# Two attention-and-MLP stages on one core: from three attention visits per unit to one, in one unrolled program

## The chip, the core and the metric

The kernel runs on one NeuronCore of a Trainium2 chip. Its engines are PE (TensorE, the matrix engine), DVE (VectorE), ACT (ScalarE), POOL (GpSimd) and SP (SyncE, which here only issues transfers). The metric is the device time in microseconds (us) of one execution; lower is better.

## The reference: what is computed

Gated linear attention over 4 batches, 8 heads, 768 tokens, head size 48, then two gated MLPs over the 3072 tokens:

```python
f = sigmoid(f_logit)
for t in range(S):                                   # S = 768
    state = f[t][:, None] * state + outer(k[t], v[t])
    y[t] = q[t] @ state
x = y as 3072 tokens x 384
x = (sigmoid(x @ w_gate) * (x @ w_val)) @ w_out      # hidden size 1536, all of it in float32
h = x @ w_in                                         # hidden size 2048
out = (h * sigmoid(1.702 * h)) @ w_out2
```

## The kernel before

**Attention in chunks.** A unit is a pair of heads of one batch over half its tokens: 384 tokens, three chunks of 128. There are 32 units. `prepare` (L480) runs the cumulative product of the gates with a scan (L487), inverts it (L491) and copies its chunk ends (L492) on DVE; `decay` (L352) multiplies q by the product (L357) and k by the inverse (L361) on POOL. PE visits each unit three times. `unit_scores` (L595) transposes k (L601) and makes the scores (L608); `unit_kv` (L612) makes the k-v products of each chunk (L618); `unit_y` (L622) multiplies scores by v (L628) and the states by q (L633). DVE masks the scores (`mask`, L495) and carries the states from chunk to chunk (`new_states`, L507: L514, then one L519 per chunk). ACT takes k (L410) and y (L415) out of PSUM. SP moves y into the MLP's input tile `x_raw` (L281). The first four units run before any MLP work.

**MLP 1.** All operands are split into a high and a low part in fp32r, and every product is three matmuls (`products`, L637: lines 640, 641, 642). Tokens go in 8 groups of 384, and hidden columns in 12 blocks of 128 (J1). A block is 9 matmuls for the gate, 9 for the value (`hidden`, L644) and 9 for the output of the block before it (`out`, L655), 27 in all of 384 columns, so 2,592 over the stage. ACT takes the sigmoid (L447), DVE multiplies (L565), ACT rounds to the high part (L453), DVE subtracts (L568). The schedule is written out by hand: the tables `Y_AT`, `SCORES_AT`, `KV_AT`, `PREPARE_AT` and `FORGET_AT` say in which block each engine puts in a step of an attention unit. The groups of batches 1 and 2 are the body of a hardware loop (`stage_a`, L214), so PE has one backward branch there; batches 0 and 3 are written out.

**Weights.** ACT's queue loads a piece of W1 of 576 KB (L393), ACT rounds it (L398), POOL subtracts (L367), each piece one block's weights. This happens in group 0. The load of piece t has to wait until POOL is through with piece t-2, which sat in the same half of `stage`. In group 0 the load of piece j+4 stands in block j ahead of ACT's rounding of piece j+3: it waits for a subtraction that POOL was given one block earlier.

**The join.** Between the MLPs all engines meet at block ends and load a flag; if a gate product had fallen below a safe bound, a slow exact path would run. It does not with these inputs, and each engine branches over it.

**MLP 2.** 6 groups of 512 tokens, 16 blocks of 18 matmuls of 512 columns (lines 1053, 1054, 1055; 1,728 in all), with its own weight splitting on ACT and DVE (L966, L1003). Its output leaves through DVE (L1017) and SP (L956).

## Time and profile before

| | |
|---|---|
| median of 3 runs | 1019.33 us (1018.74 to 1224.03) |
| the profiled execution | 1019.89 us |
| its span, first to last instruction | 1018.2 us |
| mean granted TensorE clock | 0.985 |
| PE busy | 986.6 us, 97% |
| PEld (weight loads, overlapping PE) busy | 873.7 us, 86% |
| DVE, ACT, POOL busy | 482.0, 301.2, 97.9 us |

A busy time here is the union of the instructions of an engine. Matmuls overlap one another in the records, so the pace of PE is read from the distance between the starts of two matmuls, not from their durations. The page shows PE as the only engine close to its span, and its 40 slices of the granted clock stand at nine tenths or more but for three.

### The profile page before, as it was taken

Reading aid. Unit: us, or ns where it says so; the run is one execution under the profiler, and the core shown is the slowest. Engines: PE = TensorE matmul, PEld = TensorE weight load, DVE = VectorE, ACT = ScalarE, POOL = GpSimd, SP = SyncE. Lnnn points to the kernel's source line nnn. Section 1 sums busy time; section 2 is a strip of 40 time slices with the busy share of each in tenths; the row PEclk is TensorE's granted clock in tenths of the full one; section 3 lists DMA queues with packets and bytes.
Section 4 is the critical chain, followed back from the end, with each engine's and each line's share of the span. In section 5 each row is a group of like instructions: output and inputs, shape, how many; then the busy total and the mean of one; then the engine's idle time right before and its main releaser. Section 6 shows DMA issues by size and latency. Waiting matters only on the chain. (4 is left out here: it accounts for less than half of the span.)

```text
span 1018.2 us, 15899 instructions
## 1 busy us (share of the span) xinstructions
PE 986.6 (97%) x5905; PEld 873.7 (86%) x5905; DVE 482.0 (47%) x829; ACT 301.2 (30%) x567; POOL 97.9 (10%) x88
## 2 busy tenths in 40 slices
PE   8689999999999999999999997999999999999998
PEld 5588999999999899999999995888888888888886
DVE  8566544643653554555443224654344343433433
ACT  2233322222222222222222214543233333232322
POOL 4335301110110110010010000000000000000000
PEclk9789999999999999999999998999999999999999
DMA  5434221121211211211100204311010010100000
GB/s 157 123 96 144 65 65 41 42 68 33 82 44 33 67 48 31 64 51 44 59 7 27 81 1 131 95 32 63 1 62 1 1 62 0 37 25 0 32 0 32
DMA packets 33800, 52.11 MB, mean 51 GB/s; under 512 B 6080, under 2 KB 25536, under 8 KB 33728
## 3 DMA queue, kind: packets, MB, share of 16 engines
q1 hardware_dynamic: 32000, 44.06, 14.5%
q10 hardware_dynamic: 1728, 7.08, 2.3%
q8 instruction: 46, 0.75, 0.3%
q14 instruction: 26, 0.21, 0.1%
HBM read 36.96 MB, written 9.44 MB: 46 GB/s over the span
## 5 line engine op out<-in xcount | busy, mean ns | idle before, releaser
L565 DVE TENSOR_TENSOR act_f<-act_f,value_ps 128x384 f32<-128x384 f32 x96 | 53.0, 552 | 218.5 <-PE value_ps L642 218.5
L1030 DVE TENSOR_TENSOR sil<-sil,hid_ps 128x512 f32<-128x512 f32 x96 | 66.0, 688 | 152.9 <-ACT sil L985 152.6
L1053 PE MATMUL final_ps<-sil_hi,w_hi 128*128 128x512 f32 x288 | 112.3, 390 | 1.5 <-DVE sil_lo L1033 1.5
L1053 PE MATMUL hid_ps<-x_hi,w_hi 128*128 128x512 f32 x288 | 112.9, 392 | 0.0
L1054 PE MATMUL hid_ps<-x_lo,w_hi 128*128 128x512 f32 x288 | 112.7, 391 | 0.0
L1055 PE MATMUL hid_ps<-x_hi,w_lo 128*128 128x512 f32 x288 | 112.5, 391 | 0.0
L1055 PE MATMUL final_ps<-sil_hi,w_lo 128*128 128x512 f32 x288 | 112.1, 389 | 0.0
L1054 PE MATMUL final_ps<-sil_lo,w_hi 128*128 128x512 f32 x288 | 112.0, 389 | 0.0
L985 ACT ACTIVATE sil<-hid_ps 128x512 f32<-128x512 f32 x96 | 57.5, 598 | 179.3 <-PE hid_ps L1055 179.3
L453 ACT CAST act_hi<-act_f 128x384 fp32r<-128x384 f32 x96 | 49.3, 513 | 186.9 <-DVE act_f L565 186.9
L447 ACT ACTIVATE act_f<-gate_ps 128x384 f32<-128x384 f32 x96 | 47.1, 491 | 192.4 <-PE gate_ps L642 192.4
L640 PE MATMUL gate_ps<-x_hi,w_hi 128*128 128x384 f32 x288 | 97.1, 337 | 6.4 <-DVE x_lo L526 4.6
L640 PE MATMUL out_ps<-act_hi,w_hi 128*128 128x384 f32 x288 | 102.4, 356 | 0.3 <-DVE act_lo L568 0.3
L1033 DVE TENSOR_TENSOR sil_lo<-sil,sil_hi 128x512 fp32r<-128x512 f32 x96 | 66.5, 692 | 74.4 <-ACT sil_hi L988 74.4
L640 PE MATMUL value_ps<-x_hi,w_hi 128*128 128x384 f32 x288 | 100.2, 348 | 0.0
L642 PE MATMUL value_ps<-x_hi,w_lo 128*128 128x384 f32 x288 | 97.2, 337 | 0.0
L641 PE MATMUL value_ps<-x_lo,w_hi 128*128 128x384 f32 x288 | 97.0, 337 | 0.0
L642 PE MATMUL gate_ps<-x_hi,w_lo 128*128 128x384 f32 x288 | 96.9, 336 | 0.0
L641 PE MATMUL gate_ps<-x_lo,w_hi 128*128 128x384 f32 x288 | 96.8, 336 | 0.0
L641 PE MATMUL out_ps<-act_lo,w_hi 128*128 128x384 f32 x288 | 96.6, 335 | 0.0
L642 PE MATMUL out_ps<-act_hi,w_lo 128*128 128x384 f32 x288 | 96.4, 335 | 0.0
L568 DVE TENSOR_TENSOR act_lo<-act_f,act_hi 128x384 fp32r<-128x384 f32 x96 | 54.2, 565 | 61.6 <-ACT act_hi L453 61.6
(89 smaller groups left out, 1565.5 us busy)
## 6 DMA issues: line engine op xcount, KB each, us to landing
stage<-w ACTq DMA_DIRECT2D x12, 576.0 KB, 4.0
stage<-w SPq DMA_DIRECT2D x16, 384.0 KB, 3.3
f_raw<-f_t SPq DMA_DIRECT2D x64, 72.0 KB, 2.0
k_raw<-k_t SPq DMA_DIRECT2D x64, 72.0 KB, 1.9
q_raw<-q_t SPq DMA_DIRECT2D x64, 72.0 KB, 2.0
v_raw<-v_n SPq DMA_DIRECT2D x32, 144.0 KB, 2.3
x_dram<-final SPq DMA_DIRECT2D x24, 192.0 KB, 2.0
x_in<-x_dram SPq DMA_DIRECT2D x6, 768.0 KB, 4.5
```

The costliest lines, as they stand in the source:

```text
L453: act.copy(act_hi[:, t, :], act_f[:, t, :]).then_inc(act_hi_done, 1)
L565: dve.tensor_tensor(act_f[:, t, :], act_f[:, t, :], value_ps[:, 0:GA], ALU.mult).then_inc(act_done, 1)
L568: dve.tensor_tensor(act_lo[:, t, :], act_f[:, t, :], act_hi[:, t, :].bitcast(F32), ALU.subtract).then_inc(act_split[t], 1)
L640: pe.matmul(dst, w_hi, m_hi, start=first, stop=False)
L641: pe.matmul(dst, w_hi, m_lo, start=False, stop=False)
L642: return pe.matmul(dst, w_lo, m_hi, start=False, stop=last)
L985: act.activation(sil[:, t, :], hid_ps[:, t, :], ACT.Sigmoid, scale=1.702).then_inc(b_sig_done, 1)
L1030: dve.tensor_tensor(sil[:, t, :], sil[:, t, :], hid_ps[:, t, :], ALU.mult).then_inc(sil_done, 1)
L1033: dve.tensor_tensor(sil_lo[:, t, :], sil[:, t, :], sil_hi[:, t, :].bitcast(F32), ALU.subtract).then_inc(sil_split[t], 1)
L1053: pe.matmul(dst, w_hi, m_hi, start=first, stop=False)
L1054: pe.matmul(dst, w_hi, m_lo, start=False, stop=False)
L1055: return pe.matmul(dst, w_lo, m_hi, start=False, stop=last)
```

## The change

The kernel is rewritten throughout. Chunks are 64 tokens, a unit is 256 tokens of a pair of heads (48 units), and the masks and states follow. Two chunks lie side by side on the two halves of the partitions, so the score, k-v and score-by-v matmuls have 64 rows or fewer and 64 columns or fewer and each sits on one of four 64x64 tiles of the array. One `visit` on PE does, for three successive units, the transposes and scores of one (`turned`), the k-v products of the second (`kept`) and y of the third (`made`); 52 visits, 7 of them before the MLP, 9 in group 0, 36 in groups 1 to 5. MLP 1 has groups of 256, 5 x 512 and 256 tokens. W1 and W2 share the tiles `w_hi` and `w_lo`; POOL now subtracts for both, and W2 is split during the last group of MLP 1, in stage slots filled by SP. Both MLPs are one list of blocks (`BLOCK`), without hardware loops and without a join between them; the flag is loaded and branched on at the end of the program. The multiplication of scores by v for one unit has 16 instructions of 64 columns where it had 12 of 128 for 384 tokens. The core of the diff:

```diff
-        Y_AT = {1: 0, 4: 1, 7: 2, 9: 3}, {1: 0, 3: 1, 7: 2, 9: 3}
-        SPLIT_X_AT = 10
-        SCORES_AT = {0: 0, 2: 1, 5: 2, 7: 3, 11: 4}, {1: 1, 5: 2, 7: 3, 11: 4}
-        KV_AT = {0: 0, 2: 1, 6: 2, 8: 3}, {0: 0, 2: 1, 6: 2, 8: 3}
-        PREPARE_AT = {0: 1, 3: 2, 4: 3, 9: 4, 11: 5}, {3: 2, 4: 3, 9: 4, 11: 5}
-        FORGET_AT = {2: 2, 3: 3, 8: 4, 10: 5}, {2: 2, 3: 3, 8: 4, 10: 5}
...
-        def stage_a(eng, body):
-            for h in range(HALVES):
-                body(0, h)
-            with eng.Fori(1, B - 1) as b:
-                for h in range(HALVES):
-                    body(b, h)
-            for h in range(HALVES):
-                body(B - 1, h)
...
+    W = 256
+    C = 64
+    SIDES = P // C
+    BLOCKS = W // P
+    CH = W // C
+    STEPS = TOK // W
+    THIRDS = S // W
+    UNITS = STEPS * UG
...
+    N = 512
+    GROUPS1 = [(0, W)] + [(t, N) for t in range(W, TOK - W, N)] + [(TOK - W, W)]
...
+    VISITS = [(0, None, None), (1, 0, None), (2, 1, 0), (3, 2, 1), (None, 3, 2), (None, None, 3), (4, None, None),
+              (5, 4, None)]
+    VISITS += [(n, n - 1, n - 2) for n in range(6, UNITS)] + [(None, UNITS - 1, UNITS - 2), (None, None, UNITS - 1)]
+    BEFORE_MLP = 7
...
+    VISIT_AT = {}
+    for g in range(NG1 - 1):
+        if g == 0:
+            first, js = BEFORE_MLP, range(9)
+        elif len(steps_of(g + 1)) == 2:
+            js = (0, 1, 3, 4, 5, 7, 8, 9)
+        else:
+            js = (0, 1, 3, 4)
+        for j in js:
+            VISIT_AT[g, j] = first
+            first += 1
+    assert first == len(VISITS)
+    SPLIT_AT1 = 10
+    SPLIT_AT2 = 4
...
+                def load_w2(t):
+                    if t < STAGED:
+                        sp.wait_ge(w1_split, J1)
+                    else:
+                        sp.wait_ge(w2_split, t - STAGED + 1)
+                    sp.dma_start(w2_stage[:, t % STAGED, :], w2[:, t * PIECE2:(t + 1) * PIECE2]).then_inc(w2_loaded[t % STAGED], 16)
...
+                decay(0)
+                decay(1)
+                decay(2)
+                decay(3)
+                split_w1(0)
+                decay(4)
+                split_w1(1)
+                decay(5)
+                decay(6)
...
+                for q in range(BLOCKS1):
+                    b = BLOCK[q]
+                    if (b.g, b.j) in VISIT_AT:
+                        turned, _, _ = VISITS[VISIT_AT[b.g, b.j]]
+                        if turned is not None:
+                            decay(turned + 2)
+                    if b.g == 0 and b.j + AHEAD < J1:
+                        split_w1(b.j + AHEAD)
+                for t in range(J2):
+                    split_w2(t)
...
+                def load_w1(t):
+                    wait(act, w1_split, t - 1)
+                    act.dma_start(w1_stage[:, t % 2, :], w1[:, t * PIECE1:(t + 1) * PIECE1]).then_inc(w1_loaded[t % 2], 16)
+                def w1_first_part(t):
+                    act.wait_ge(w1_loaded[t % 2], 16 * (t // 2 + 1))
+                    act.copy(w_hi[:, t * PIECE1:(t + 1) * PIECE1], w1_stage[:, t % 2, :]).then_inc(w1_hi_done, 1)
...
+                    act.wait_ge(w2_loaded[t % STAGED], 16 * (t // STAGED + 1))
+                    act.wait_ge(act_used, BLOCKS1 - J1 + w2_free_at[t])
+                    act.copy(w_hi[:, t * PIECE2:(t + 1) * PIECE2], w2_stage[:, t % STAGED, :]).then_inc(w2_hi_done, 1)
...
+                load_w1(0)
+                load_w1(1)
+                forget(0)
+                forget(1)
+                take_k(0)
+                forget(2)
+                take_k(1)
+                w1_first_part(0)
+                forget(3)
+                take_y(0)
+                take_k(2)
+                load_w1(2)
+                take_y(1)
+                take_k(3)
+                forget(4)
+                w1_first_part(1)
+                take_y(2)
+                take_y(3)
+                forget(5)
+                take_k(4)
+                load_w1(3)
+                x_first_part(0)
+                forget(6)
+                forget(7)
...
+                    act.wait_ge(mul_done, q + 1)
+                    wait(act, act_used, q - 1)
+                    act.copy(act_hi[:, b.t, 0:b.n], act_f[:, b.t, 0:b.n]).then_inc(act_hi_done, 1)
+                    if b.first_mlp and (b.g, b.j) in VISIT_AT:
+                        turned, _, made = VISITS[VISIT_AT[b.g, b.j]]
+                        if turned is not None:
+                            take_k(turned)
+                        if made is not None:
+                            take_y(made)
+                        if turned is not None:
+                            forget(turned + 3)
+                    if b.first_mlp and b.g == 0:
+                        if b.j + AHEAD < J1:
+                            w1_first_part(b.j + AHEAD)
+                        if b.j + AHEAD + 2 < J1:
+                            load_w1(b.j + AHEAD + 2)
...
+                    dve.tensor_tensor_scan(prod[:, u.s, :], gate[:, u.s, :], floor[:, u.s, :], 1.0, ALU.mult,
+                                           ALU.max).then_inc(scan_done, 1)
+                    dve.wait_ge(scan_done, n + 1)
+                    wait(dve, k_dec_done, n - 1)
+                    dve.reciprocal(inv_prod[:, u.s, :], prod[:, u.s, :]).then_inc(inv_done, 1)
+                    dve.tensor_copy(p_end[:, n, :],
+                                    prod[:, u.s, :].rearrange("p (c t) -> p c t", c=CH)[:, :, C - 1]).then_inc(p_end_done, 1)
...
+                    dve.wait_ge(kv_done, n + 1)
+                    for m, c in enumerate(range(0 if u.third else 1, CH)):
+                        if m:
+                            dve.wait_ge(state_done, states_before(n) + m)
+                        dve.scalar_tensor_tensor(out=after[:, c, :], in0=state_before(u, c), scalar=p_end[:, n, c:c + 1],
+                                                 in1=after[:, c, :], op0=ALU.mult, op1=ALU.add).then_inc(state_done, 1)
+                def after_visit(v):
+                    turned, kept, made = VISITS[v]
+                    dve.wait_ge(visit_done, v + 1)
+                    if made is not None:
+                        dve.wait_ge(y_taken, made + 1)
+                    if turned is not None:
+                        mask(turned)
+                    if kept is not None:
+                        new_states(kept)
...
+                dve.wait_ge(gaps_set, 6)
+                prepare(0)
+                prepare(1)
+                after_visit(0)
+                prepare(2)
+                after_visit(1)
+                prepare(3)
+                after_visit(2)
+                after_visit(3)
+                after_visit(4)
+                dve.wait_ge(visit_done, 6)
+                prepare(4)
+                x_second_part(0)
+                prepare(5)
+                after_visit(6)
+                prepare(6)
...
+                    dve.wait_ge(act_hi_done, q + 1)
+                    dve.tensor_tensor(act_lo[:, b.t, 0:b.n], act_f[:, b.t, 0:b.n], act_hi[:, b.t, 0:b.n].bitcast(F32),
+                                      ALU.subtract).then_inc(act_split, 1)
+                    v = VISIT_AT.get((b.g, b.j)) if b.first_mlp else None
+                    if v is not None:
+                        after_visit(v)
+                    if b.j == 0 and b.group:
+                        take_out(b.group - 1)
+                    if v is not None and VISITS[v][0] is not None:
+                        prepare(VISITS[v][0] + 2)
...
+                def visit(v):
+                    turned, kept, made = VISITS[v]
+                    if turned is not None:
+                        u = Unit(turned)
+                        pe.wait_ge(k_dec_done, turned + 1)
+                        wait(pe, k_rows_done, turned)
+                        for c in range(BLOCKS):
+                            at = slice(c * P, (c + 1) * P)
+                            last = pe.transpose(turn_ps[:, at], k_dec[:, u.s, at], ident[:, :])
+                        last.then_inc(k_turned, 1)
+                    if v:
+                        before = VISITS[v - 1]
+                        if before[0] is not None:
+                            pe.wait_ge(scores_masked, before[0] + 1)
+                        if before[1] is not None:
+                            pe.wait_ge(kv_done, before[1] + 1)
+                        if before[2] is not None:
+                            pe.wait_ge(y_taken, before[2] + 1)
+                    opens = True
+                    if made is not None:
+                        m = Unit(made)
+                        pe.wait_ge(scores_masked, made + 1)
+                        for c in range(BLOCKS):
+                            at = slice(Y_COL + c * C, Y_COL + (c + 1) * C)
+                            for r in range(SIDES):
+                                for i in range(PAIR):
+                                    last = pe.matmul(att_ps[rows[i], r, at], v_raw[halves[r], made % 4, c, cols[i]],
+                                              scores[halves[r], made % 2, i, c, :], start=opens and c == 0, stop=False,
+                                              skip_group_check=True)
+                        opens = False
...
+                    if turned is not None:
+                        pe.wait_ge(q_dec_done, turned + 1)
+                        for c in range(BLOCKS):
+                            for i in range(PAIR):
+                                for r in range(SIDES):
+                                    at = slice(c * P + r * C, c * P + (r + 1) * C)
+                                    last = pe.matmul(att_ps[halves[r], i, c * C:(c + 1) * C], k_dec[rows[i], u.s, at],
+                                                     q_dec[rows[i], turned % 4, at], start=opens and c == 0, stop=False,
+                                                     skip_group_check=True)
+                    if made is not None:
+                        last.then_inc(tiles_done, 1)
+                        pe.wait_ge(tiles_done, made + 1)
+                        pe.wait_ge(state_done, states_before(made + 1))
+                        for c in range(0 if m.third else 1, CH):
+                            at = slice(Y_COL + c // SIDES * C, Y_COL + (c // SIDES + 1) * C)
+                            for i in range(PAIR):
+                                last = pe.matmul(att_ps[rows[i], c % SIDES, at], state_before(m, c)[rows[i], :],
+                                                 q_dec[rows[i], made % 4, c * C:(c + 1) * C], start=False, stop=False,
+                                                 skip_group_check=True)
+                    last.then_inc(visit_done, 1)
...
+                for v in range(BEFORE_MLP):
+                    visit(v)
+                    keep_warm({1: 3, 2: 3, 3: 2, 5: 6, 6: 6}.get(v, 0))
+                for b in BLOCK:
+                    q = b.q
+                    if b.first_mlp:
+                        if b.g == 0:
+                            pe.wait_ge(w1_split, b.j + 1)
+                        wait(pe, sig_done, q)
+                        hidden(b, 0, b.j * PIECE1, gate_ready)
+                        wait(pe, mul_done, q)
+                        hidden(b, 1, b.j * PIECE1 + KC * P, value_ready)
+                        if (b.g, b.j) in VISIT_AT:
+                            visit(VISIT_AT[b.g, b.j])
...
+                    if q:
+                        out(BLOCK[q - 1])
+                out(BLOCK[-1])
...
+                redo = unsafe_value(pe)
+                with pe.If(redo):
+                    columns(pe, r_column)
```

## Rows read from the trace of the kernel before

**Rows 1.** The page's first part: busy time, share of the span, instructions of each engine.
```profile
PE 986.6 (97%) x5905; PEld 873.7 (86%) x5905; DVE 482.0 (47%) x829; ACT 301.2 (30%) x567; POOL 97.9 (10%) x88
```

**Rows 2.** The timeline of PE, MLP 1 and a scores visit: start us, us, instructions.
```profile
400.78 0.33 PE L640 MATMUL gate_ps<-x_hi,w_hi 128*128 128x384 f32 x1
...
408.41 0.34 PE L642 MATMUL value_ps<-x_hi,w_lo 128*128 128x384 f32 x1
408.58 0.49 PE L601 MATMUL att_ps<-ident,k_dec 128*128 128x128 f32 x3
409.00 0.94 PE L608 MATMUL att_ps<-q_dec,k_dec 48*128 48x128 f32 x12
409.87 0.44 PE L640 MATMUL out_ps<-act_hi,w_hi 128*128 128x384 f32 x1
410.15 0.34 PE L641 MATMUL out_ps<-act_lo,w_hi 128*128 128x384 f32 x1
```

**Rows 3.** The same timeline, a k-v visit.
```profile
414.49 0.34 PE L642 MATMUL value_ps<-x_hi,w_lo 128*128 128x384 f32 x1
414.76 0.56 PE L618 MATMUL att_ps<-v_raw,k_rows 128*64 128x48 f32 x12
415.24 0.45 PE L640 MATMUL out_ps<-act_hi,w_hi 128*128 128x384 f32 x1
```

**Rows 4.** The same timeline, a y visit.
```profile
418.30 0.34 PE L642 MATMUL gate_ps<-x_hi,w_lo 128*128 128x384 f32 x1
...
419.93 0.44 PE L640 MATMUL value_ps<-x_hi,w_hi 128*128 128x384 f32 x1
```

**Rows 5.** The same timeline: the loop's branch, the join, MLP 2 from start to end.
```profile
340.24 0.44 PE L640 MATMUL gate_ps<-x_hi,w_hi 128*128 128x384 f32 x1 [1.79 <-issue]
...
617.39 2.05 PE L1086 MATMUL hid_ps<-stage 128*128 128x128 f32 x8 [6.68 <-PEq L756]
...
625.97 0.50 PE L1053 MATMUL final_ps<-sil_hi,w_hi 128*128 128x512 f32 x1 [0.70 <-DVE sil_lo L1033]
...
1011.44 0.39 PE L1055 MATMUL final_ps<-sil_hi,w_lo 128*128 128x512 f32 x1
...
1014.54 0.40 PE L1055 MATMUL final_ps<-sil_hi,w_lo 128*128 128x512 f32 x1
```

**Rows 6.** The same timeline: the first matmul of MLP 1.
```profile
45.00 0.66 PE L640 MATMUL gate_ps<-x_hi,w_hi 128*128 128x384 f32 x1 [4.64 <-DVE x_lo L526]
```

**Rows 7.** The timeline of DVE, ACT and POOL in group 0.
```profile
91.69 0.55 DVE L565 TENSOR_TENSOR act_f<-act_f,value_ps 128x384 f32<-128x384 f32 x1 [2.35 <-PE value_ps L642]
92.28 0.51 ACT L453 CAST act_hi<-act_f 128x384 fp32r<-128x384 f32 x1 [1.73 <-DVE act_f L565]
92.29 0.33 ACTq L393 DMA_DIRECT2D stage<-w  x1
92.70 1.15 ACT L398 CAST w_hi<-stage 128x1152 fp32r<-128x1152 f32 x1
...
93.59 3.05 DVE L519 SCALAR_TENSOR_TENSOR state<-state,p_end 128x48 f32<-128x48 f32 x2
93.93 2.65 POOL L367 TENSOR_TENSOR w_lo<-stage,w_hi 128x1152 fp32r<-128x1152 f32 x1 [2.54 <-ACT w_hi L398]
```

**Rows 8.** The timeline of DVE in the first 16 us: one unit's mask and states.
```profile
12.69 1.01 DVE L502 TENSOR_TENSOR scores<-att_ps,causal 128x384 f32<-128x384 f32 x2
13.62 0.30 DVE L514 TENSOR_TENSOR state<-att_ps,p_end 128x144 f32<-128x144 f32 x1
13.95 0.57 DVE L519 SCALAR_TENSOR_TENSOR state<-state,p_end 128x48 f32<-128x48 f32 x2
```

**Rows 9.** Groups by line: operation, shapes, count, busy us, mean ns, idle before.
```profile
L491 DVE RECIPROCAL inv_prod<-prod 128x384 f32<-128x384 f32 x32 | 81.7, 2553 | 1.1
...
L487 DVE TENSOR_TENSOR_SCAN prod<-gate,floor 128x128 f32<-128x128 f32 x96 | 34.4, 414 | 1.8 <-ACT gate L404 1.6
L361 POOL TENSOR_TENSOR k_dec<-k_raw,inv_prod 128x384 f32<-128x384 f32 x32 | 32.3, 1010 | 44.7 <-issue 41.8 <-DVE inv_prod L491 2.9
```

More of the change, by code:

```diff
@@ L725, in gla_moe_moe2 @@
         r_stored = sem("r_stored")
[L726 to L735 removed]
+        CONSTS = 2
@@ new lines, in gla_moe_moe2, with pieces_of_head @@
+        rows = [slice(64 * i, 64 * i + D) for i in range(PAIR)]
+        halves = [slice(64 * i, 64 * i + 64) for i in range(PAIR)]
+        cols = [slice(D * i, D * i + D) for i in range(PAIR)]
+        def pieces_of_head(head):
+            at, end = head * D, head * D + D
+            while at < end:
+                rows_here = min(end, (at // P + 1) * P) - at
+                yield at - head * D, at // P, at % P, rows_here
+                at += rows_here
+        MOVES = [sum(len(list(pieces_of_head(PAIR * p + i))) for i in range(PAIR)) for p in range(UG)]
@@ L844, in _, with keep_warm @@
             @block.tensor
             def _(pe):
-                def inside(n, b, p, e):
+                def keep_warm(times):
+                    for _ in range(times):
+                        pe.matmul(up_ps[:, 0, 0:P], ident[:, :], ident[:, :], start=True, stop=True)
+                pe.wait_ge(warm_set, 1)
+                for _ in range(8):
+                    pe.matmul(up_ps[:, 0, 0:384], x_raw[:, 0, 0:P], x_raw[:, 0, 0:384], start=True, stop=True)
+                pe.wait_ge(consts_set, CONSTS)
```

1261 lines of the change are left out of this document (501 added, 760 removed).

## The prediction

> **What bounds the kernel now.** The first part of the page comes first: PE is busy for 97% of the span, no other engine for half of it [rows 1]. The pace of PE then comes from the timeline. In MLP 1, 44 distances from 400.78 to 408.41 make 0.1733 us for one matmul of 384 columns [rows 2]; in MLP 2, 1,700 distances from 625.97 to 1011.44 make 0.2267 us for 512 [rows 5]. The difference for 128 columns is 0.053 us, which is the 2.4 GHz clock, so each matmul pays about 0.013 us beyond its columns. 2,592 x 0.1733 = 449.2 us and 1,728 x 0.2267 = 391.7 us: the MLPs are 841 us of 1,018.
>
> The rest, in order of time: 45.0 us before the first MLP matmul [rows 6]; the attention visits; a branch; the join; the tail. A visit's price is the distance between the MLP matmuls around it less 0.173, plus 0.11 because the next one is late as well (0.28 from 409.87 to 410.15 in place of 0.17) [rows 2]. Scores: 1.46 - 0.17 + 0.11 = 1.40 us. K-v: 0.75 - 0.17 + 0.11 = 0.69 [rows 3]. Y: 1.63 - 0.17 + 0.11 = 1.57 [rows 4]. The two halves of a batch differ by about 0.1, and a unit costs about 3.7 us; 28 units lie inside the MLP, 104 us. The loop's branch costs 2.0 us, the join 6.7 us of idle PE and then 2.1 us of warm-up and 1.7 us of slow matmuls before 625.97 [rows 5]. 45.0 + 449.2 + 104 + 2.0 leaves about 10 us of MLP 1 that are waits and a halved clock in group 0. From the last matmul at 1014.54 to the end of the span are 3.6 us [rows 5].
>
> **The change, part by part.** I put the new program together in order of time.
>
> *Matmuls.* Groups of 512: 5 x 324 x 0.2267 = 367.2 us. Groups of 256: 106.7 ns of columns and 0.013 are 0.120 us each, 324 x 0.120 = 38.9 us a group. A bound from below is 0.107; from above 0.130, if the weight load does not quite hide. MLP 2 stays at 391.7.
>
> *A visit.* The two transposes cost 0.107 us each, and the step from them into small tiles 0.20 (409.00 - 408.58 = 0.42 for three transposes with that step) [rows 2]. A float32 matmul is two instructions. The 12 k-v instructions, 48 columns each against 64 columns of weights, run two at a time on two column tiles: 0.48 us with 0.13 to 0.2 of the way back, so six rounds of 0.05 to 0.06 us; I take 0.058 [rows 3]. No row shows four tiles at once. If four go as two do, the 48 instructions of scores, k-v and scores-by-v take 12 rounds of 0.058: 0.70 us. If only two go at a time, it is 24 rounds, 1.40 us. I take the first, because pairs by rows (L608) and by columns (L618) both ran side by side [rows 2, 3]. Then the new wait: PE waits for its own tiles before it adds the states' part, about 0.35 us. The 16 instructions with the states sit on two tiles only: 8 rounds, 0.46. Back to the MLP 0.20, and 0.11. The sum is 0.11 + 0.20 + 0.70 + 0.35 + 0.46 + 0.20 + 0.11 = 2.13 us, or 2.83. One unit in three has 4 fewer state instructions (0.12). Groups 1 to 5 hold 36 visits: 36 x 2.13 - 1.4 = 75.3 us. Per token of a head pair, 2.1 us per 256 against 3.7 per 384 is 14% less, because three switches became one, but states and waits stay.
>
> A rule speaks against this gain. The Trainium skill, "TensorE: Matmul & The Clock Gate", section "Wait — 56ns, not 53.3ns?", gives a start-to-start floor of about 25 ns for any matmul. By it the 48 instructions would take 1.2 us and the kernel 18 us more; k-v's 12 in some 0.35 us, 29 ns each [rows 3], neither break the floor nor prove it.
>
> *Before the MLP.* DVE sets the order. A unit of 256 costs it: scan 2/3 of 1.05, reciprocal 2/3 of 2.553 = 1.70, chain-end copy 0.1, so `prepare` is 2.5 us [rows 9]; mask 0.33 (two of 384 take 1.01) and states 0.38 + 4 x 0.30, so `after_visit` is 1.9 us [rows 8]. The chain prepare(0), visit and after_visit of units 0 to 3 ends near 28 us. Then ACT's list holds up `x_first_part(0)` behind `load_w1(3)`, which waits for POOL's subtraction of piece 1, which POOL does after decay(4), after prepare(4): 28.2 + 2.5 + 0.8 + 2.65 + 0.4 = 34.5. The first MLP matmul comes about 1 us later, at 35.5, against 45.0.
>
> *Group 0.* This is the step that I think decides. In block j ACT rounds piece j+2 and at once waits, to load piece j+4, for POOL's subtraction of piece j+2. POOL has decay(turned+2) ahead of that, and this needs DVE's `prepare`, which comes behind `after_visit`. Behind ACT's wait stands the sigmoid of block j+1, and DVE's product waits for it. So DVE, POOL and ACT run one after another: after_visit 1.9; prepare up to the inverse 2.47; k's decay 0.15 + 0.74 (1.010 for 384 columns) [rows 9]; subtraction 2.6; load issue 0.4 with its wait; sigmoid 0.4; product 0.5; rounding 0.5; k and y out of PSUM and the signal 0.75 [rows 7]. That is 10.4 us a block, for blocks 0 to 7, where PE has 27 x 0.120 + 2.13 = 5.4 us of work. The kernel before asks for the load one block earlier and has no such ring. From 35.5: 7.5 us to the first after_visit in the group (prepare(5), mask, prepare(6), product), 8 x 10.4 = 83.2, blocks 8 to 11 14.5, slow clock 1.3. Group 1 starts at 142.0 us; with PE alone as the bound it would be 94.
>
> DVE's states wait for POOL: two of L519 take 3.05 us beside a subtraction [rows 7] and 0.57 without [rows 8]. In the ring they never meet, so it costs nothing there. The Trainium skill, "SBUF — State Buffer", section "🔬 SBUF: two separate sides", makes this a lock against every DVE instruction with two SBUF inputs; the row agrees.
>
> *Groups 1 to 5* run at PE's pace: DVE's chain per block is 0.7 + 0.6 + 0.7 + 0.7 (take k and y) + 1.9 + 2.5 = 7.1 us beside 27 x 0.2267 + 2.13 = 8.25. If the cover were gone, it would be the excess times 36. 36 x 2.13 is counted above.
>
> *Group 6 and W2.* SP fills three slots; ACT, then POOL (about 1.8 us a piece) split 1.5 pieces in a block of 3.24 us. POOL is nearly full, DVE's subtraction has to get in between, and a load of some 4 us comes every three pieces. Nothing or 10 us; I take 4.
>
> *Tail.* One wait of the last block, 1.0; 3.6 as now; and the flag and branch at the end. At the join a taken branch kept PE idle for most of 6.7 us [rows 5]. Beside the last stores I take 3, between 0 and 6.
>
> *Hand-over* between the MLPs and the loop's branch: nothing is left of them, 10 and 2 us gone.
>
> **Sum.** 142.0 + 367.2 + 38.9 + 75.3 + 4 + 391.7 + 1.0 + 3.6 + 3 = 1026.7 us of span. The profiled execution has 1019.89 for a span of 1018.2, so 1.7 more: **1028 us**. Its own time is 0.6 above the median of 1019.33. The gains (about 10 before the MLP, 12 of join and branch, 5 of fewer matmuls, 14 of visits) are eaten by group 0 (48 of wait for the 10 now), W2 and the tail.
>
> **Rivals.** *The ring does not close*, because a wait that I place last has long been met. Then group 0 goes by DVE and POOL under their lock, about 7.3 us a block: 8 x 3.1 = 25 us less, and 4 with W2 hidden, so 999. With PE alone as the bound everywhere: 1028 - 48 - 4 = 976. For it: the ring before was open and lost only 10 us. Against: the order of the lists, which I can read. Chance 0.24, two thirds of it beyond 2%.
>
> *Four tiles do not run at once.* Place: the three tile groups of each visit in groups 1 to 5; price 0.70 us x 36 = 25, so 1053, slower. It decides from 0.45 us a visit on (16 us). For it: no instruction of the trace has more than two beside each other, and none starts on average less than 29 ns after the last [rows 3]. Against: rounds are set by weight loading, per tile. The skill's floor is the same rival at 1046. Chance 0.24.
>
> *The change does less than it says*: POOL's lock and DVE's order put waits into the visits of groups 1 to 5 as well, 1 us for each, 36: 1064. Chance 0.06. My forecast has the remaining 0.46, with its own range of 1012 to 1042.
>
> **How the numbers follow.** About 2% is what a measurement of this kernel can tell from no change: 999 to 1040. Faster by more: 0.16 of the first rival and 0.01 of the forecast, 0.17. Slower: 0.21 + 0.05 + 0.03 = 0.29. Within: 0.54. The range 997 to 1056 leaves out the PE-bound end of the first rival and most of the third.
>
> **What would show it.** After the change, PE's distances should be 0.2267 and 0.120 us; a full visit 2.0 to 2.3 us between MLP matmuls; the first MLP matmul at 35 us. In group 0, ACT's sigmoids should stand about 10 us apart, each just behind a 576 KB load issued at the end of a POOL subtraction, DVE idle until ACT's sigmoid, PE about half busy with a lower granted clock. The forecast is wrong if the sigmoids stand 6 to 7 us apart, or if a visit takes 2.8. PE should show no gap where MLP 2 begins but small ones in group 6, and a longer tail than 3.6 us.

## The result and the profile after

The changed kernel took 1028.35 us (median of 4 runs, 1026.85 to 1029.57), beside 1019.04 for the kernel before on the same chip. The ratio is 1.0095, with a 95% interval of 1.0075 to 1.0114: nearly 1% slower, inside the 2% that stand for no change, and 0.35 us from the 1028 that was forecast. The profiled execution took 1026.85 us, its span is 1025.1, against 1018.2 before, so the spans differ by 6.9 us. One run of the kernel before took 1224.03 us; the ratio leaves it out.

The page's first part after, for [rows 1]:

```profile
PE 966.2 (94%) x7157; PEld 803.2 (78%) x7157; DVE 486.2 (47%) x864; ACT 303.4 (30%) x620; POOL 133.5 (13%) x134
```

PE has 20 us less of busy time than before and yet a span that is 7 us longer: the change did save TensorE work, and about 27 us went into waiting. The page's slices say where (40 slices of 25.6 us; a digit is a share in tenths, in the second line the granted clock):

```profile
PE   6767589999999999999999999899999999999997
PEclk8778899999999999999999999999999999999999
```

Apart from one 8, near 640 us, everything under 9 ahead of the last slice lies in the first six slices, up to 154 us, which are the part before the MLP and group 0. A timeline of PE from the middle of group 1 (start us, duration us, instructions) shows one visit and the pace around it, for [rows 2 to 4]:

```profile
182.17 0.39 PE L911 MATMUL up_ps<-x_hi,w_lo 128*128 128x512 f32 x1
...
183.53 0.39 PE L911 MATMUL up_ps<-x_hi,w_lo 128*128 128x512 f32 x1
183.76 0.38 PE L849 MATMUL turn_ps<-ident,k_dec 128*128 128x128 f32 x2
184.07 0.44 PE L869 MATMUL att_ps<-scores,v_raw 64*48 64x64 f32 x16
184.33 0.40 PE L881 MATMUL att_ps<-v_raw,k_rows 64*64 64x48 f32 x16
184.55 0.43 PE L891 MATMUL att_ps<-q_dec,k_dec 48*64 48x64 f32 x16
185.07 0.65 PE L902 MATMUL att_ps<-q_dec,state 48*48 48x64 f32 x16
185.65 0.50 PE L909 MATMUL out_ps<-act_hi,w_hi 128*128 128x512 f32 x1
185.99 0.40 PE L910 MATMUL out_ps<-act_lo,w_hi 128*128 128x512 f32 x1
```

Six distances from 182.17 to 183.53 make 0.227 us, as in MLP 2 before. The visit lies between 183.53 and 185.65: 2.12 - 0.23 + 0.11 (the next distance is 0.34) = 2.00 us, where 2.13 was put down. The 22 visits of groups 1 to 5 that transpose and have 16 instructions with the states cost 2.00 each, the 12 with 12 such instructions 1.89 or less. The tile groups start 0.26 and 0.22 us apart, 16 instructions each, which is the price taken for four tiles at once. The other length of matmul has its pace at the start of group 6, where three distances from 579.73 to 580.09 make 0.12 us.

Group 0 is the place that decides. This is the timeline of the other engines over one block there, from one sigmoid to the next; a bracket gives the idle time before an instruction and what ended it. It answers to [rows 7]:

```profile
83.81 0.38 ACT L583 ACTIVATE act_f<-up_ps 128x256 f32<-128x256 f32 x1 [6.86 <-POOL w_lo L462]
84.22 0.42 DVE L762 TENSOR_TENSOR act_f<-act_f,up_ps 128x256 f32<-128x256 f32 x1 [4.31 <-ACT act_f L583]
...
86.45 1.18 DVE L700 SCALAR_TENSOR_TENSOR state<-state,p_end 128x48 f32<-128x48 f32 x4
...
88.27 1.75 DVE L674 RECIPROCAL inv_prod<-prod 128x256 f32<-128x256 f32 x1
...
90.16 0.72 POOL L456 TENSOR_TENSOR k_dec<-k_raw,inv_prod 128x256 f32<-128x256 f32 x1 [1.05 <-issue]
90.84 2.61 POOL L462 TENSOR_TENSOR w_lo<-stage,w_hi 128x1152 fp32r<-128x1152 f32 x1
93.47 0.34 ACTq L498 DMA_DIRECT2D stage<-w  x1
93.91 0.38 ACT L583 ACTIVATE act_f<-up_ps 128x256 f32<-128x256 f32 x1 [6.83 <-POOL w_lo L462]
```

Read it as a ring: each instruction begins where one on another engine ends. ScalarE stands 6.8 us for GpSimd's subtraction, issues the load and only then makes the sigmoid; VectorE stands 4.3 us for the sigmoid; and the subtraction at 90.84 hangs on VectorE's reciprocal. One turn is 93.91 - 83.81 = 10.10 us. From block 1 on the sigmoids of group 0 start at 53.5, 63.6, 73.7, 83.8, 93.9, 104.1, 114.2 and 124.3. Group 1's first matmul starts at 142.36. Wherever a run is said below to start group 1, its tenth matmul is meant, which starts at 144.43 here. The view of waits over the whole span has two lines of it (us in total, times, longest):

```profile
ACT act_f L583 <- POOL w_lo L462: 54.2, 8, 6.9
DVE act_f L762 <- ACT act_f L583: 40.3, 11, 4.3
```

Now the stages. In the changed kernel the last nine output matmuls of a group run behind the first nine matmuls of the next one; here they are counted with their own group, so that group 0 ends at 142.36 + 9 x 0.12 = 143.4 and MLP 1 at 621.51 + 9 x 0.12 = 622.6. The first matmul of the MLP came 6.9 us sooner (38.1 for 45.0). MLP 1 ran from there to 610.7 before, 565.7 us, and to 622.6 now, 584.5: 18.8 more. Join and MLP 2 took 403.8 us to 1014.54 and now take 397.5 to 1020.05, 6.3 less. The tail is 5.0 for 3.6, 1.4 more. Together that is 7.0. Within MLP 1 the matmuls are 4 us less (5 x 324 x 0.227 + 2 x 324 x 0.12 = 445 for 449), 45 visits at most 2.0 us each take 90 or a little less for 104, and the branch of 2 is gone. So some 20 us are saved, and the waits, with the slow clock that goes with them, grew by about 40. Group 0 alone, 105.4 us, has 324 x 0.12 + 9 x 2.0 = 56.9 of work in it.

Behind group 0 stands one more hole, in MLP 2, that nothing in the prediction speaks of. DVE's and PE's timeline there:

```profile
647.58 0.27 PE L957 MATMUL turn_ps<-ident,least 128*1 128x128 f32 x1
647.89 0.28 DVE L735 TENSOR_REDUCE least<-turn_ps 1x1 f32<-1x128 f32 x1 [3.50 <-PE turn_ps L957]
...
648.45 0.67 DVE L765 TENSOR_TENSOR act_f<-act_f,up_ps 128x512 f32<-128x512 f32 x1
...
650.54 0.79 PE L909 MATMUL out_ps<-act_hi,w_hi 128*128 128x512 f32 x1 [2.69 <-DVE act_lo L769]
```

`flag()` reduces the chunks' last products on VectorE, waits for TensorE's transpose of them, and reduces again. The transpose stands two blocks further down in TensorE's order, so VectorE waits 3.50 us in it, and the product of the block behind it is late: TensorE waits 2.69, and five of its next distances are 0.43 us in place of 0.23, at the lower clock (0.83 granted from 645 to 655 us).

### The profile page after: what moved, and what is told of

Its sections match the earlier page's. It is cut to its first block, busy times and chain, and to the rows that moved or that the text cites. A ratio compares the mean times of both kernels' runs of the same rounds, so it can differ in the third digit from the quotient of the medians.

```text
span 1025.1 us, 17700 instructions
## 1 busy us (share of the span) xinstructions
PE 966.2 (94%) x7157; PEld 803.2 (78%) x7157; DVE 486.2 (47%) x864; ACT 303.4 (30%) x620; POOL 133.5 (13%) x134
## 4 chain that ended last, share of the span: by engine, by line
PE 83%; DVE 2%; ACT 1%; POOL 1%; issue 1%; DMA 0%; ACTq 0%; DVEq 0%
PE up_ps L909 15%; PE up_ps L911 15%; PE up_ps L910 15%; PE out_ps L909 11%; PE out_ps L911 11%; PE out_ps L910 11%; PE att_ps L902 2%; PE att_ps L869 1%; PE att_ps L891 1%; PE att_ps L881 1%; PE turn_ps L849 1%; DVE act_lo L769 0%; POOL w_lo L469 0%; DMA stage<-w 0%; DVE x_lo L717 0%
## 5 line engine op out<-in xcount | busy, mean ns | idle before, releaser
L909 PE MATMUL up_ps<-x_hi,w_hi 128*128 128x512 f32 (+1 forms) x792 | 299.1, 378 | 34.5 <-ACT act_f L583 28.5
L911 PE MATMUL up_ps<-x_hi,w_lo 128*128 128x512 f32 (+1 forms) x792 | 297.2, 375 | 0.0
L910 PE MATMUL up_ps<-x_lo,w_hi 128*128 128x512 f32 (+1 forms) x792 | 297.1, 375 | 0.0
L909 PE MATMUL out_ps<-act_hi,w_hi 128*128 128x512 f32 (+1 forms) x540 | 208.5, 386 | 4.2 <-DVE act_lo L769 4.0
L911 PE MATMUL out_ps<-act_hi,w_lo 128*128 128x512 f32 (+1 forms) x540 | 203.4, 377 | 0.0
L910 PE MATMUL out_ps<-act_lo,w_hi 128*128 128x512 f32 (+1 forms) x540 | 203.1, 376 | 0.0
L909 PEld LDWEIGHTS up_ps<-x_hi,w_hi 128*128 128x128 f32 x792 | 153.7, 194 | 61.9 <-POOL w_lo L462 34.8
L769 DVE TENSOR_TENSOR act_lo<-act_f,act_hi 128x512 fp32r<-128x512 f32 (+1 forms) x180 | 123.1, 684 | 118.5 <-ACT act_hi L589 118.5
L589 ACT CAST act_hi<-act_f 128x512 fp32r<-128x512 f32 (+1 forms) x180 | 106.5, 592 | 237.1 <-DVE act_f L762 160.5
L910 PEld LDWEIGHTS up_ps<-x_lo,w_hi 128*128 128x128 f32 x792 | 154.0, 194 | 25.4
L911 PEld LDWEIGHTS up_ps<-x_hi,w_lo 128*128 128x128 f32 x792 | 153.7, 194 | 25.5
```

What stands on the lines that cost most here:

```text
L589: act.copy(act_hi[:, b.t, 0:b.n], act_f[:, b.t, 0:b.n]).then_inc(act_hi_done, 1)
L769: dve.tensor_tensor(act_lo[:, b.t, 0:b.n], act_f[:, b.t, 0:b.n], act_hi[:, b.t, 0:b.n].bitcast(F32), ALU.subtract).then_inc(act_split, 1)
L909: pe.matmul(dst, w_hi[:, at:at + P], m_hi, start=first, stop=False)
L910: pe.matmul(dst, w_hi[:, at:at + P], m_lo, start=False, stop=False)
L911: return pe.matmul(dst, w_lo[:, at:at + P], m_hi, start=False, stop=last)
```

## The experiments

The forecast's theory was the ring in group 0. Its rivals for the missing time were a price of the visits, and VectorE and GpSimd as the bound of group 0 by their own work. All times below are medians; the kernel before took 1018.5 us beside the first four kernels, 1018.1 beside the next four and 1017.4 beside the last two.

**Ask for the load one block later in program order, ahead of the rounding.**

```diff
                     if b.first_mlp and b.g == 0:
+                        if b.j and b.j + AHEAD + 1 < J1:
+                            load_w1(b.j + AHEAD + 1)
                         if b.j + AHEAD < J1:
                             w1_first_part(b.j + AHEAD)
-                        if b.j + AHEAD + 2 < J1:
-                            load_w1(b.j + AHEAD + 2)
```

> The load of piece j+3 is asked for in block j ahead of the rounding of piece j+2 (in the changed kernel: the load of piece j+4 right behind that rounding), so it waits for a subtraction that POOL was given one block earlier. Theory of the ring (DVE's prepare, POOL's decay and subtraction, ACT's load and sigmoid follow one another because ACT waits for the youngest subtraction): the sigmoids of group 0, 10.1 us apart in the changed kernel, come to 6.5 to 7.5 us, the limit of DVE and POOL with their exclusive pairs of instructions; 8 x 3 = 24 us less, about 1004 us. Rival (DVE's and POOL's own work with their waits on each other sets the block time, the load's place is chance): the sigmoids stay above 9.5 us, and the time falls by less than 5 us.

Measured: 1004.64 us (1003.04 to 1005.09), ratio to before 0.9865 (0.9848 to 0.9882). The sigmoids of group 0 stand 7.1 us apart from 84.6 us on, between 5.1 and 8.7 before that, and group 1 starts at 121.4, 23.0 us sooner; the time fell by 23.7. One line's place in ScalarE's list made the difference between 1% slower and 1.3% faster, and nothing of the arithmetic moved. The ring is shown, and so is its price. What is left shows in the timeline of VectorE and GpSimd:

```profile
80.26 2.88 POOL L462 TENSOR_TENSOR w_lo<-stage,w_hi 128x1152 fp32r<-128x1152 f32 x1
81.58 2.54 DVE L700 SCALAR_TENSOR_TENSOR state<-state,p_end 128x48 f32<-128x48 f32 x4
```

With the ring open, the two engines meet: the four state updates take 2.54 us instead of 1.18, and the subtraction 2.88 instead of 2.61. The first update alone takes 1.62 and ends at 83.20, where the subtraction ends at 83.14; the three behind it take their usual 0.27 each.

**GpSimd subtracts before it decays, in the ring as it was.**

```diff
+                    if b.g == 0 and b.j + AHEAD < J1:
+                        split_w1(b.j + AHEAD)
                     if (b.g, b.j) in VISIT_AT:
                         ...
                             decay(turned + 2)
-                    if b.g == 0 and b.j + AHEAD < J1:
-                        split_w1(b.j + AHEAD)
```

> Only POOL's order in group 0 changes: the subtraction of the weight piece ahead of the decay. Theory of the ring: ACT still waits for the youngest subtraction, but this no longer waits for DVE's prepare and k's decay. It starts about 1.9 us after after_visit begins and holds up DVE's scan for about 2.6 us; the sigmoid follows beside the reciprocal. The block time falls from 10.1 to about 8.8 us, the time by about 10 us to 1018. If the load's place were not in the ring, the order on POOL would change nothing or make it longer, since DVE's scan has to wait: 1028 or more.

Measured: 1007.76 us (1005.36 to 1009.78), ratio 0.9905 (0.9887 to 0.9923). The direction is right and the size is wrong: it gained 20.6 us, twice what was expected. The sigmoids stand 6.5 and 8.5 to 8.9 us apart, mostly by turns, 7.8 on the average. The long blocks are the 8.8 us that were expected; the short ones were not. This edit takes VectorE's states and reciprocal out of the ring, since the subtraction no longer stands behind a decay that needs them. ScalarE still waits for the subtraction in every block, 3.2 to 3.6 us for 6.8, but in the short blocks TensorE does not wait for the sigmoid.

**The order of the small matmuls, tile by tile.** The loops over the three tile groups of a visit were turned inside out, so that two neighbouring matmuls of the list go to the same tile, where the list went round the tiles before (for y: `for r`, `for i`, then `for c`, in place of `for c`, `for r`, `for i`).

> In a visit the block of tokens is now the innermost loop of the scores, k-v and scores-by-v matmuls, so that two matmuls of one tile (four instructions) follow each other before the next tile. If PE starts work for free tiles ahead of what waits for a busy one, nothing changes: a visit's gap stays 2.12 us and 16 instructions take 0.23 us. If PE takes instructions in their order and four tiles ran together only because the order went round the tiles, 16 instructions take 3 to 4 times as long, the gap becomes 3.5 us or more and the time rises by over 40 us. In between (a short look ahead): 2.4 to 3.0 us.

Measured: 1028.26 us in a single run, span 1026.5. The same kind of visit as above on PE's timeline:

```profile
184.25 0.46 PE L869 MATMUL att_ps<-scores,v_raw 64*48 64x64 f32 x16
184.51 0.43 PE L881 MATMUL att_ps<-v_raw,k_rows 64*64 64x48 f32 x14
184.73 0.23 PE L891 MATMUL att_ps<-q_dec,k_dec 48*64 48x64 f32 x1
184.74 0.23 PE L881 MATMUL att_ps<-v_raw,k_rows 64*64 64x48 f32 x2
184.78 0.46 PE L891 MATMUL att_ps<-q_dec,k_dec 48*64 48x64 f32 x15
185.32 0.65 PE L902 MATMUL att_ps<-q_dec,state 48*48 48x64 f32 x16
```

The groups start 0.26 and 0.22 us apart, as before the edit; only the part behind them comes 0.08 us later. One scores instruction starts ahead of the last two of k-v. So the order in the list matters little.

**The flag in two parts.** VectorE makes the first reduction where it was, and the other three instructions three blocks later, when the transpose is long done.

```diff
                     dve.tensor_reduce(least[:, 0:1], ...).then_inc(least_done, 1)
+                def flag_rest():
                     dve.wait_ge(least_done, 2)
...
                     if b.group == NG1 and b.j == SPLIT_AT2:
                         flag()
+                    if b.group == NG1 and b.j == SPLIT_AT2 + 3:
+                        flag_rest()
```

> DVE's flag is split: the minimum over the gate products stays behind block 4 of the first group of MLP 2, the part that needs PE's transpose comes behind block 7, and PE's transpose stays in block 6. In the changed kernel DVE stands 3.5 us before that transpose with the products of block 5 behind it, PE then waits 2.7 us for them and runs 6 matmuls at 1.2 GHz. Theory: all of it goes, 2.9 us of waiting and about 1.5 us of slow clock, 4.4 us less, 1024 us. Rival (PE would have waited there for ACT and DVE anyway): less than 1 us.

Measured: 1024.03 us (1023.78 to 1025.05), ratio 1.0061 (1.0045 to 1.0078), 4.3 us under the changed kernel. After the first reduction, which ends near 645.9, VectorE's next product starts without a wait:

```profile
645.61 0.34 DVE L733 TENSOR_REDUCE least<-p_end 128x1 f32<-128x192 f32 x1
645.89 0.69 DVE L767 TENSOR_TENSOR act_f<-act_f,up_ps 128x512 f32<-128x512 f32 x1
```

From the first matmul of MLP 2 to the end of the span the profiled run is 4.6 us shorter than the changed kernel's. That is the whole of the hole and of the slow matmuls behind it.

**ScalarE splits x before it asks for piece 3.** The first MLP matmul came at 38.07 in place of 35.5. In ScalarE's prologue `x_first_part(0)` waited 1.95 us behind `load_w1(3)`, so the two lines were exchanged, in the changed kernel.

> The changed kernel with one edit, x_first_part(0) ahead of load_w1(3) in ScalarE's prologue. The first MLP matmul comes 1.9 us earlier (36.2 us). If the start counts in full, 1028.35 - 1.9 = 1026.5. If the ring of group 0 takes it back (piece 3 is asked for no earlier, and every later piece hangs on it), group 1 starts at 144.4 as before and the time stays 1028.3.

Measured: 1026.01 us (1025.29 to 1026.86), ratio 1.0078 (1.0061 to 1.0095); the profiled span is 1025.1, as it was, and the rounding came 1.8 us earlier. Yet the first matmul did not:

```profile
34.21 2.62 POOL L462 TENSOR_TENSOR w_lo<-stage,w_hi 128x1152 fp32r<-128x1152 f32 x1
...
35.30 1.02 ACT L549 CAST x_hi<-x_raw 128x256 fp32r<-128x256 f32 x3
35.56 2.93 PE L834 MATMUL up_ps<-ident 128*128 128x128 f32 x12
35.74 2.04 DVE L717 TENSOR_TENSOR x_lo<-x_raw,x_hi 128x256 fp32r<-128x256 f32 x3 [2.33 <-ACT x_hi L549]
...
38.14 0.56 PE L909 MATMUL up_ps<-x_hi,w_hi 128*128 128x256 f32 x1
```

Two things stood behind the wait that was taken away: the kernel's own warm-up matmuls keep TensorE until 38.1, and VectorE's `x_lo`, 1.09 us for three in the changed kernel, takes 2.04 beside GpSimd's subtraction. Both my readings of this place were too short. Group 1 starts at 144.24 for 144.43. The medians are 2.3 us apart, but the intervals of the two ratios overlap and the two profiled spans are equal, so no gain is shown.

**The three edits together.** Load order, flag and prologue.

> Three edits at once: the load order of the first run (load_w1(j+3) ahead of w1_first_part(j+2)), the flag in two parts, and in ScalarE's prologue x_first_part(0) ahead of load_w1(3), which waits for GpSimd's second subtraction. If the three waits are independent terms of the path, the gains add: 1004.6 of the first run, less 4.3 (the flag), less 1.9 (ScalarE's wait at 33.9 to 36.6 us, so that the first matmul of the MLP starts at about 36.2 instead of 38.1), so 998.4 us. Rival: the start of the MLP is not what paces group 0, the ring is, and what is won ahead of it is waited away by the block that uses piece 3: then group 1 starts where it did in the first run (121.4) and the time is 1000.3.

Measured: 1001.2 us (997.44 to 1001.45), ratio 0.9824 (0.9801 to 0.9848). The rival's 1000.3 is nearer than 998.4, but the time alone does not choose between them (its interval is about 997.8 to 1002.6); the trace does. From the tenth matmul of MLP 2, at 602.4, to the end the profiled run is 4.4 us shorter than with the load order alone, which is the flag, while group 1 starts at 123.0, 1.6 later than there. So nothing is left of the sooner start. Where it is lost was not tested; the trace shows four `act_lo` of group 0 lengthened beside GpSimd, where the load order alone has two. One of them, which takes 0.42 when GpSimd rests:

```profile
87.01 2.62 POOL L462 TENSOR_TENSOR w_lo<-stage,w_hi 128x1152 fp32r<-128x1152 f32 x1
...
88.08 1.83 DVE L771 TENSOR_TENSOR act_lo<-act_f,act_hi 128x256 fp32r<-128x256 f32 x1 [0.47 <-ACT act_hi L589]
```

**The three edits, and GpSimd subtracts first.** The edit of the second experiment on top of them.

> The three edits and, on GpSimd, the subtraction ahead of the two decay multiplications. In the first run the sigmoids of group 0 stand 7.1 us apart on the average where a block with its visit would need 36 x 0.120 + 2.0 = 6.3. If GpSimd's order is what is left, blocks come down to about 6.5 and the time falls by 8 x 0.6 = 4.8 to 993.6. If what is left is elsewhere (VectorE's row of work, 5.3 us and lengthened beside GpSimd), the order changes nothing or costs (decay later, so the next visit's transposes later): 998 to 1001.

Measured: 1002.38 us (1001.9 to 1003.1), ratio 0.9851 (0.9834 to 0.9867): no gain, the blocks are 7.9 to 8.2 us long. The gains of the first and second experiment do not add, because both open the same ring; and now the subtraction, here from 69.80 to 72.44, falls upon the states:

```profile
69.09 3.41 DVE L700 SCALAR_TENSOR_TENSOR state<-state,p_end 128x48 f32<-128x48 f32 x4
...
72.65 0.65 PE L906 MATMUL att_ps<-q_dec,state 48*48 48x64 f32 x16 [2.58 <-DVE state L700]
```

Four updates of 0.3 us take 3.41, and TensorE stands 2.58 us in the middle of a visit for them.

**VectorE subtracts W1's pieces 2 to 11.** On top of the three edits, `split_w1` of group 0 goes from GpSimd's list to VectorE's, behind the states.

```diff
 (GpSimd)
-                    if b.g == 0 and b.j + AHEAD < J1:
-                        split_w1(b.j + AHEAD)
 (VectorE, behind after_visit)
+                    if b.first_mlp and b.g == 0 and b.j + AHEAD < J1:
+                        split_w1(b.j + AHEAD)
```

> The three edits, and pieces 2 to 11 of W1's subtraction moved from GpSimd to VectorE, behind the states of the visit. By 0.552 us for 384 columns in the kernel before a piece takes VectorE about 1.6 us where GpSimd took 2.6; VectorE's work of a block of group 0 is 5.3 us (0.42 + 0.42 + 0.41 + 0.34 + 1.18 + 0.68 + 1.75 + 0.11), so 6.9 with it. If GpSimd's subtraction beside VectorE's two-input work was what stretched both (VectorE rows of 1.85 to 2.2 us where 0.42 is usual), these stretches go and a block takes about 7.0 us with VectorE as its bound: the time is that of the three edits within 2 us, 996 to 1000. If VectorE had room, 990 to 994. If its longer row of work delays act_lo and the mask, over 1003.

Measured: 994.59 us (993.96 to 995.2), ratio 0.9774 (0.9757 to 0.979). This is faster than both kernels, by 2.3% than the one before and by 3.2% than the changed one (0.9774 / 1.0095). The timeline of VectorE in group 0:

```profile
81.47 1.35 DVE L708 TENSOR_TENSOR w_lo<-stage,w_hi 128x1152 fp32r<-128x1152 f32 x1
...
83.46 1.75 DVE L676 RECIPROCAL inv_prod<-prod 128x256 f32<-128x256 f32 x1
...
85.15 0.41 DVE L772 TENSOR_TENSOR act_f<-act_f,up_ps 128x256 f32<-128x256 f32 x1
```

The four state updates ahead of these rows take 1.18 us, the piece 1.35 us for GpSimd's 2.6, and VectorE runs from one row into the next: it is the bound, at 7.1 us a block, as expected. The time is 1.4 us under the 996 to 1000 expected; the piece was put down at 1.6 us, and ten of them at 0.25 us less are 2.5 us, which is enough for that. The windows view from 45 to 115 us (busy us of PE, PEld, VectorE, ScalarE and GpSimd with their counts, then the granted clock, the DMA share and GB/s) shows the three stages of the repair, the changed kernel, the load order alone, and this one:

```profile
45.00:115.00 70.00, 44.02 (x642) 39.57 (x641) 34.79 (x77) 18.88 (x47) 28.26 (x22) 0.85 0.37 100
```
```profile
45.00:115.00 70.00, 51.79 (x780) 46.99 (x779) 55.14 (x100) 27.19 (x63) 41.04 (x28) 0.91 0.45 130
```
```profile
45.00:115.00 70.00, 54.07 (x812) 48.77 (x811) 59.47 (x112) 27.69 (x67) 13.19 (x18) 0.98 0.46 129
```

VectorE's busy time in the same 70 us goes from 35 to 59, TensorE does 812 instructions where it did 642, and its clock comes up from 0.85 to 0.98 with them. In the first line no engine is near full, which is how a ring looks in a table of busy times: not one busy engine, but three that take turns.

**VectorE subtracts W2's pieces too.** In the kernel above, 43.0 us lie between the tenth matmul of group 6 and the tenth of MLP 2, and `act_lo` takes up to 2.1 us there. I set 38.9 against the 43.0, the pace of 324 matmuls of 256 columns. But 18 of the matmuls between these two have 512 columns, so their pace is 306 x 0.12 + 18 x 0.227 = 40.8, and 2.2 us are lost, not 4.1.

> The kernel with W1's subtraction on VectorE (994.6 us), and W2's sixteen subtractions moved from GpSimd to VectorE too, in the block in which ScalarE rounds the piece. In group 6 of that kernel 324 matmuls take 43.0 us where 38.9 is their pace; VectorE's act_lo takes 1.0 to 2.1 us there beside GpSimd's 1.85 us subtractions, where 0.42 is usual. If this stretching is what group 6 loses, VectorE (0.85 us a block of its own and 0.9 for a piece, by 1.35 for 1152 columns) has room in a block of 3.24 us for one piece but hardly for two: group 6 takes 40 to 41 us and the time is 992 to 993. If the loads of the pieces are what it loses, group 6 stays at 43. Rival: in the blocks with two pieces VectorE waits for ScalarE's rounding of both and the next product is late: group 6 over 44, the time over 996.

Measured: 993.72 us (991.95 to 995.67), ratio 0.9777 (0.9759 to 0.9796), no difference to the one before it. Between the same two matmuls lie 42.4 us, so 1.6 us are lost where it was 2.2; the expected 40 to 41 rested on the short pace. Where the kernel above had

```profile
568.27 1.49 DVE L779 TENSOR_TENSOR act_lo<-act_f,act_hi 128x256 fp32r<-128x256 f32 x1 [0.47 <-ACT act_hi L591]
569.69 3.54 DVE L725 TENSOR_TENSOR x_lo<-x_raw,x_hi 128x512 fp32r<-128x512 f32 x3
```

this one has

```profile
568.50 1.66 ACT L549 CAST x_hi<-x_raw 128x512 fp32r<-128x512 f32 x3
570.06 0.83 ACT L510 CAST w_hi<-stage 128x768 fp32r<-128x768 f32 x1
...
570.92 0.96 DVE L712 TENSOR_TENSOR w_lo<-stage,w_hi 128x768 fp32r<-128x768 f32 x1 [1.87 <-ACT w_hi L510]
571.80 1.89 DVE L729 TENSOR_TENSOR x_lo<-x_raw,x_hi 128x512 fp32r<-128x512 f32 x3
```

The stretching is gone (`x_lo` 1.89 for 3.54), and VectorE waits 1.87 us for a piece that is not rounded yet. The load is not to blame: ScalarE rounds the three parts of x and then, without an idle time, the piece, and over the whole run it waits 0.3 us for loads of W2. One wait took the other's place.

**Without the last warm-up matmuls.**

> The kernel with W1's subtraction on VectorE (994.6 us), without the six warm-up matmuls (12 instructions) between visit 6 and the first matmul of the MLP. They run from 35.0 to 37.6 us, and VectorE's x_lo, three in 2.05 us beside GpSimd's subtraction, has its first part ready near 35.9. If the warm-up is what holds the MLP's start, the first matmul comes at 36.0 to 36.5; the first ones run at 1.2 GHz, 36 matmuls at 0.21 at the worst in place of 0.12. Group 0 is then paced by VectorE's row of work (7.1 us a block), which does not start earlier, so group 1 starts at 115.9 as before, within 0.7: no change of the time. If the start counts in full, -1.3 us. If the clock stays low for longer, +2 to +3.

Measured: 995.74 us (994.5 to 997.15), ratio 0.9792 (0.9776 to 0.9807), the same or 1 us more than with them. The first MLP matmul comes at 36.90 for 37.61, bound by `x_lo`, of which three take 2.28 us beside GpSimd's subtraction:

```profile
36.90 0.36 PE L923 MATMUL up_ps<-x_hi,w_hi 128*128 128x256 f32 x1 [2.11 <-DVE x_lo L725]
```

and group 1 starts at 117.1 for 115.9, 0.4 us beyond the 0.7 that was allowed; the first matmuls run at a lower granted clock, 0.81 from 36 to 45 us for 0.86. The start of the MLP is worth nothing as long as group 0 is paced by something else.

## Why the prediction was right

The time was right to 0.35 us, and the mechanism, the ring of ScalarE, GpSimd and VectorE in group 0, was the right one. The mechanism was read; the 0.35 us is luck, as the steps show (each group with its own output matmuls, as above):

- **Matmul pace.** 0.227 and 0.120 us were predicted and measured.
- **Visits.** 2.00 us for 2.13. The transposes and the switch take 0.31 as put down (183.76 to 184.07), the 48 instructions and the wait for PE's own tiles 1.00 for 1.05, the states and the way back 0.58 for 0.66. That makes groups 1 to 5 438.1 us for 442.5, 4.4 less, which is what the 36 visits are cheaper by. The rival of two tiles at a time is ruled out, and so is the third, of waits in these visits: 2.00 and 1.89 leave no room for them.
- **A rule that was weighed.** Sixteen instructions start in 0.22 to 0.26 us, 14 to 16 ns each, so that the 48 take about 0.7 us and not the 1.2 that the rule would make. The floor of about 25 ns for any matmul that the Trainium skill gives ("TensorE: Matmul & The Clock Gate", "Wait — 56ns, not 53.3ns?") does not hold across tiles here.
- **The first MLP matmul.** 38.1 for 35.5, and the span has 2.6 us more here. VectorE begins `prepare(4)` at 30.63, where the sum had 28.2, and from there on the steps are about as long as put down. The states wait for GpSimd's subtraction of piece 0 there, the meeting that the prediction had read in the kernel before and looked for in the ring alone:

```profile
20.49 2.61 POOL L462 TENSOR_TENSOR w_lo<-stage,w_hi 128x1152 fp32r<-128x1152 f32 x1
20.64 3.14 DVE L700 SCALAR_TENSOR_TENSOR state<-state,p_end 128x48 f32<-128x48 f32 x3
```

  Three updates take 0.87 us elsewhere, so 2.3 us are lost in this row, and TensorE waits 2.06 us for it; no run takes it away. I also left out the warm-up matmuls on TensorE, which the exchanged lines in ScalarE's prologue then ran into.
- **The ring.** 10.1 us a block for 10.4, and group 0 took 105.4 for 106.5. The experiment that opened it gave back 23.7 us where the first rival was priced at 25.
- **GpSimd and VectorE.** That they would never meet inside the ring is right: the states take 1.18 us there. That they meet once it is open keeps the first repair above the last: with VectorE doing both, the time is 994.6 where 1001.2 stood. The Trainium skill ("SBUF — State Buffer", "🔬 SBUF: two separate sides") calls it an exclusive lock between a VectorE instruction with two SBUF inputs and a GpSimd instruction that reads SBUF; the rows of 3.41, 2.54, 2.04 and 1.83 us agree. With the subtraction on VectorE none is lengthened from 45 to 115 us.
- **Group 6.** 41.0 us, 2.2 of excess for the 4 taken. Of the two causes that the prediction names it was VectorE's lengthened work: TensorE's two holes in the changed kernel (0.94 and 0.60 us of idle time) stand behind an `x_lo` of 2.33 us and an `act_lo` of 2.08. Taking the lengthening away left 1.6 us, and these go to the order of ScalarE's and VectorE's lists, not to the loads.
- **MLP 2.** 397.5 for 392.7, the largest error of the sum. This step failed: `flag()` was listed in the tail and its wait in the middle of VectorE's work was not looked for. It costs 4.3 us.
- **Tail.** 5.0 for 6.6; the branch costs 1.4 us at most where 3 was taken.

The errors of +2.6 (start), -1.1 (group 0), -4.4 (groups 1 to 5), -1.9 (group 6), +4.8 (MLP 2) and -1.6 (tail) cancel to -1.6, the difference between the span of 1025.1 and the sum of 1026.7. The total is nearer than its parts deserve, but the term that carries the sign is right by itself. The gain that one might expect of this change was real, some 20 us in MLP 1 and 13 around it; it went into a load request that stands behind a wait in ScalarE's list.

Still open is which part of VectorE's 7.1 us a block could be moved on to ScalarE, and why the blocks of the second repair alternate between 6.5 and 8.8 us.

## What to carry to other kernels

When a rewrite changes how often an engine must wait per block, write down for one block the order of each engine's list and follow every wait to the engine that ends it. If the path comes back to where it began, its length is the block's time, whatever the busy shares say, and the cheapest repair is to move one request ahead of, or behind, one instruction. Then look at what the freed engines will meet: here an open ring brought GpSimd and VectorE together, and the larger gain came from giving the work to one of them.

## What the runs showed that I had not expected

- The rewrite leaves 34 us that the order and place of existing work decide: 994.6 us with four such edits, and the same arithmetic.
- VectorE subtracts 1152 columns in 1.35 us, less than three times its 0.56 for 384 (`act_lo` in the kernel before), and half of GpSimd's 2.6.
- In the kernel with the tile order turned round, a matmul of one tile started before earlier ones of another (184.73 before 184.74), so by the records the starts do not keep to the order of the list across tiles.
- Repairs of one ring do not add: 23.7 us and 20.6 us alone, and with both (beside the flag and the prologue) 1002.4 us, where 1001.2 was reached without the second.
